# Cluster scores with the tokens stationary and the 16 centroids moving, written straight in token order

## The chip, the cores and the metric

One NeuronCore of a Trainium2 chip runs the whole program. The time is the device time of that core for one launch, in microseconds; the kernel before was run three times: 958.29, 959.78 and 960.33 us, median 959.78 us. All profile rows below come from one profiled execution of it.

## The reference

Three stages, in fp32. The change is in the first.

```python
q_n = q / (norm(q) + 1e-6); k_n, c_n the same            # B=2, H=8, S=768, D=64
q_assign = argmax(einsum('bhsd,hcd->bhsc', q_n, c_n), -1)  # 16 centroids per head
k_assign = argmax(einsum('bhsd,hcd->bhsc', k_n, c_n), -1)
mask = q_assign[..., :, None] == k_assign[..., None, :]
scores = where(mask, q @ k.T / sqrt(D), -1e9)
attn = softmax(scores); x = (attn @ v) -> (1536, 512)
x = moe(x)        # top-1 of 8 experts, 512 -> 1024 -> 512, gated
out = moe2(x)     # 512 -> 2048 -> 512 with a clamped square
```

The length of a token does not change its argmax, so the kernel scores unnormalised tokens against normalised centroids. To keep fp32 accuracy with matmuls in the faster fp32r form, an operand is split into a high part (fp32r) and a low part (the rest).

## The kernel before, in words

The 16 heads (2 x 8, called 0 to 15) run one after the other through a software pipeline; each head has 6 tiles of 128 queries and 6 of 128 keys. Every engine has its own program in fixed order (blocks `block.tensor`, `block.scalar`, `block.vector`, `block.gpsimd`, `block.sync`), and semaphores tie them together; no scheduler moves anything. On each engine `attend(h)` has six steps `s` = 0 to 5. Heads 0 and 1 get their operands in a prologue before the first `attend`; for a head h+2 they are made inside `attend(h)`.

For one head, in the order of the data:

- GpSimd writes each token twice side by side (L355, `dup`), TensorE transposes the tiles into PSUM (`operands`, L1059), ScalarE copies them to `qk_t` as high parts (L499), VectorE writes the low parts (L733 for q, L738 for k). `qk_t` has four groups of six tiles: A1 (q high, in both halves of the partitions), A2 (q low in partitions 0 to 63), B1 (k: high above, low below), B2.
- GpSimd copies the head's centroids from `cen_t` to `cst` (`place_centroids`, L373 and L374).
- **Cluster scores** (`cluster_scores`, L1063 to L1074): `cst` is the stationary side, 64 columns wide, of which 16 hold centroids and the others zeros; 384 tokens move. Eight matmuls add up into one 64x384 PSUM area, whose partitions are (k or q, first or second half of the tiles, centroid). Rows alternate between 128 and 64.
- ScalarE copies this to SBUF (`copy_cluster_scores`, L513, 64x384), and TensorE transposes it back in three 128x128 pieces (`cluster_rows`, L1079), so that tokens are partitions and the scores of a token lie in its row.
- VectorE takes the maximum (L747), compares (L752), turns the comparison into a label (L758, L763) and the labels into one-hot rows (L769).
- TensorE transposes the one-hots (`onehots`, L1088), and ScalarE writes them to partitions 64 to 79 of A2 and B2 (L507). They make the mask part of the score matmul L1104.

Then come the score matmuls (L1103, L1104), row maximum (L780), exponential (L518), transposes of the probabilities (L1117), their high and low copies (L544 on ScalarE, L830 on VectorE), the product with v (L1131, L1133), and the transposes of the outputs (L1145) which VectorE normalises (L806).

TensorE does `cluster_scores(h + 2)` at step 5 of `attend(h)`, ahead of that step's probability transposes, and `cluster_rows(h + 2)` behind them. VectorE does L747 and L752 at step 5, L758 at its end, L763 and L769 at step 0 of `attend(h + 1)`; TensorE wants the one-hots in step 1 of `attend(h + 1)`. While it runs the attention, GpSimd has little to do; behind it come four large subtractions for the first expert's weights (L342).

Of the kernel before, what the change touches and what calls it, by code (L numbers as in the profile page):

```python
# [26 lines left out]
F32 = mybir.dt.float32  # L27
F32R = mybir.dt.float32r
# [7 lines left out]
P = 128  # L36
BANK = 512
B, H, S, D = 2, 8, 768, 64
NC = 16
BH = B * H  # L40
QT = S // P
# [35 lines left out]
def build(nc, q, k, v, centroids, w_gate, w_ogate, w1, w2, w_in, w_out, out):  # L77
# [8 lines left out]
    def place(name, shape, dt, at=None):  # L86
        size = 4 if dt != BF16 else 2
        for n in shape[1:]:
            size *= n
        size = -(-size // 32) * 32  # L90
        if at is None:
            at, cursor[0] = cursor[0], cursor[0] + size
        else:
            at[0], at = at[0] + size, at[0]
        return nc.alloc_sbuf_tensor_at(name, list(shape), dt, offset=at)
# [55 lines left out]
    cst = place("cst", [P, 2, 4, 6 * NC], F32R, small)  # L151
    ct_sb = place("ct_sb", [P, GW], F32, small)
# [37 lines left out]
    with ctx:  # L190
        ps = ctx.enter_context(nc.psum_tensor("ps", [P, 8, BANK], F32))

        def sem(name):
            return ctx.enter_context(nc.semaphore(name))
# [14 lines left out]
        ct_done, ct_copied, cs_done, cl_done = sem("ct_done"), sem("ct_copied"), sem("cs_done"), sem("cl_done")  # L209
# [33 lines left out]
        cs_ps = ps[:, 7, 0:GW].rearrange("p (t n) -> p t n", n=P)[:, :, 0:4 * NC]\  # L243
            .rearrange("p t (a c) -> p t a c", c=NC)
        ct_ps = ps[0:4 * NC, 7, 0:GW]
# [65 lines left out]
        def _(pool):  # L311
# [56 lines left out]
            def place_centroids(h, u):  # L368

                if h >= 2:  # L370
                    pool.wait_ge(ct_done, h - 1)
                c = slice(h % H * NC, (h % H + 1) * NC)
                pool.tensor_copy(cst[:, u, 0:2, 2 * NC:3 * NC], cen_t[:, 0:2, c])  # L373
                pool.tensor_copy(cst[:, u, 2:4, 3 * NC:4 * NC], cen_t[:, 1:3, c]).then_inc(cst_done, 1)  # L374
# [113 lines left out]
        def _(act):  # L488
# [22 lines left out]
            def copy_cluster_scores(h):  # L511
                act.wait_ge(ct_done, h + 1)
                act.activation(ct_sb[0:4 * NC], ct_ps, ACT.Copy).then_inc(ct_copied, 1)  # L513

# [14 lines left out]
            def attend(h, u, first, ahead):  # L529
                un = 1 - u  # L530
                for s in range(QT):
# [3 lines left out]
                    if s == 5 and ahead >= 2:  # L535
                        copy_cluster_scores(h + 2)
# [23 lines left out]
            copy_cluster_scores(0)  # L560
# [8 lines left out]
            copy_cluster_scores(1)  # L569
# [119 lines left out]
        def _(dve):  # L689
            dve.memset(onehot[:], 0.0)  # L690
            dve.memset(x_sb[:, :, :, DM:], 0.0)
# [26 lines left out]
            dve.memset(ct_sb[4 * NC:], 0.0)  # L718
# [321 lines left out]
        def _(pe):  # L1040
# [22 lines left out]
            def cluster_scores(h, u):  # L1063


                pe.wait_ge(opd_done, 4 * h + 4)
                pe.wait_ge(cst_done, h + 1)
                for a in range(2):
                    cols = slice(2 * NC * (1 - a), 2 * NC * (1 - a) + 4 * NC)
                    for j, (rows, t) in enumerate(((P, A1), (D, A2), (P, B1), (D, B1))):  # L1070
                        tiles = qk_t[0:rows, u, t + a * HALF:t + (a + 1) * HALF, :].rearrange("p t n -> p (t n)")
                        last = mm(ct_ps, cst[0:rows, u, j, cols], tiles, start=(a == 0 and j == 0),  # L1072
                                  stop=(a == 1 and j == 3))
                last.then_inc(ct_done, 1)  # L1074

            def cluster_rows(h):
                pe.wait_ge(ct_copied, h + 1)
                for t in range(HALF):
                    last = tr(x_ps[:, t * P:(t + 1) * P], ct_sb[:, t * P:(t + 1) * P], ident[:])  # L1079
                last.then_inc(cs_done, 1)  # L1080
# [68 lines left out]
            def attend(h, u, first, ahead):  # L1149
                un = 1 - u  # L1150
                for s in range(QT):
# [8 lines left out]
                    if s == 5 and ahead >= 2:  # L1160
                        cluster_rows(h + 2)
# [28 lines left out]
            cluster_rows(0)  # L1190
# [9 lines left out]
            cluster_rows(1)  # L1200
# [189 lines left out]
```

## Time and profile before

| | |
|---|---|
| runs | 958.29, 959.78, 960.33 us |
| span of the profiled execution, first to last instruction | 959.3 us |
| prologue of the attention (to the first `attend`) | about 38 us |
| one head in the steady loop | 20.66 us |
| attention ends | about 367 us |
| TensorE busy | 853.2 us, 89% |
| VectorE, ScalarE, GpSimd busy | 543.7, 382.0, 320.2 us |

The profiled execution's own time is its span of 959.3 us and what lies around it, and this agrees with the runs to within 1 us. The time of a head is the distance of two cluster score blocks in the chain of waits (219.81 less 199.15). "PE" in the rows is TensorE's matmul side, "PEld" its load of the stationary side, DVE VectorE, ACT ScalarE, POOL GpSimd. A line of the timeline gives start and length of a group of equal instructions; in brackets how long the engine was idle before it and who ended that. The chain of waits goes back from the last instruction of the program and names what each moment of the span was waiting for. The matmul clock is shown as a share of 2.4 GHz, so that 0.50 is 1.2 GHz.

### The profile page before, as it was taken

The numbers are of one execution on the slowest core, as the hardware profiler recorded it, in microseconds if no ns is written. First come the engines' busy times: TensorE is split into PE (matmuls) and PEld (weight loads), VectorE is DVE, ScalarE is ACT, GpSimd is POOL, SyncE is SP. The second block draws the span as 40 slices with busy tenths as digits, with TensorE's granted clock in tenths as the row PEclk, the third lists the DMA queues.
The fourth block names the chain that finished last, engine by engine and source line by source line (L and its number), as shares of the span: only waits on it lengthen the run. The fifth ranks groups of instructions, "written<-read, shape, count | busy, mean of one in ns | idle before, by whom it ended". The sixth has DMA issues, their size and how long they took to land.

```text
span 959.3 us, 13920 instructions
## 1 busy us (share of the span) xinstructions
PE 853.2 (89%) x4379; PEld 691.9 (72%) x4380; DVE 543.7 (57%) x862; ACT 382.0 (40%) x762; POOL 320.2 (33%) x302
## 2 busy tenths in 40 slices
PE   4899999999999973389997997999699999999995
PEld 2687777777777762278776876877588888888884
DVE  4487787787778786134445345343744544454442
ACT  2577677777677751021211221122122332232222
POOL 4222222222322274448874664666400010001001
PEclk9799999999999997599999999999899999999998
DMA  8000000100000065698996696786300010001001
GB/s 269 25 26 25 26 25 25 49 25 25 25 25 8 0 219 181 217 261 264 329 339 240 206 332 218 230 319 219 99 1 0 1 45 1 1 1 44 1 1 44
DMA packets 46388, 105.23 MB, mean 110 GB/s; under 512 B 6545, under 2 KB 12689, under 8 KB 45329
## 3 DMA queue, kind: packets, MB, share of 16 engines
q1 hardware_dynamic: 24656, 51.48, 16.0%
q0 software_dynamic: 17408, 48.26, 15.0%
q10 hardware_dynamic: 4288, 5.03, 1.9%
q8 instruction: 20, 0.33, 0.1%
q14 instruction: 16, 0.12, 0.0%
HBM read 98.45 MB, written 6.32 MB: 109 GB/s over the span
## 4 chain that ended last, share of the span: by engine, by line
PE 70%; DVE 13%; DMA 6%; issue 5%; ACT 3%; POOL 2%; DVEq 1%; ACTq 1%
PE ps L1343 14%; PE ps L1330 14%; PE ps L1290 8%; PE ps L1270 7%; PE ps L1117 5%; DMA x_in<-sorted_rows 5%; PE ps L1072 4%; DVE coef L962 4%; PE ps L1103 3%; PE ps L1133 2%; PE ps L1104 2%; PE ps L1145 2%; PE ps L1131 2%; PE ps L1059 2%; PE ps L1088 2%
## 5 line engine op out<-in xcount | busy, mean ns | idle before, releaser
L342 POOL TENSOR_TENSOR weights<-staging,weights 128x2048 fp32r<-128x2048 f32 x38 | 174.9, 4612 | 38.4 <-DMA weights<-in_moe_w 30.2
L1343 PE MATMUL ps<-weights,g_t 128*128 128x512 f32 x576 | 145.0, 401 | 9.0 <-DVE g_t L1033 9.0
L1330 PE MATMUL ps<-y_t,weights 128*128 128x512 f32 x576 | 141.5, 395 | 0.0
L1343 PEld LDWEIGHTS ps<-weights,g_t 128*128 128x128 f32 x576 | 108.7, 190 | 35.9 <-DVE g_t L1033 10.1
L1330 PEld LDWEIGHTS ps<-y_t,weights 128*128 128x128 f32 x576 | 108.2, 188 | 25.7
L1290 PE MATMUL ps<-weights,h_t 128*128 x456 | 114.5, 409 | 3.9 <-issue 3.8
L830 DVE TENSOR_TENSOR p_t<-ps,p_t 128x384 fp32r<-128x384 f32 x192 | 99.9, 548 | 31.4 <-ACT p_t L544 30.2
L1270 PE MATMUL ps<-weights,x_t 128*128 x456 | 111.3, 401 | 2.0 <-DVE x_t L956 1.7
L1290 PEld LDWEIGHTS ps<-weights,h_t 128*128 128x128 f32 x456 | 87.9, 196 | 24.6 <-issue 6.0
L1270 PEld LDWEIGHTS ps<-weights,x_t 128*128 128x128 f32 x456 | 85.6, 191 | 20.6 <-issue 2.6
L480 POOL DMA_INDIRECT out<-y_sb,token_u x12 | 11.9, 995 | 255.8 <-ACT y_sb L676 253.6
L780 DVE TENSOR_REDUCE nmax<-ps 128x1 f32<-128x768 f32 x96 | 90.9, 946 | 6.4 <-PE ps L1104 5.3
L544 ACT ACTIVATE p_t<-ps 128x384 fp32r<-128x384 f32 x192 | 84.0, 490 | 22.2 <-PE ps L1117 21.3
L662 ACT ACTIVATE g_a<-g_a,half 128x512 f32<-128x512 f32 x48 | 34.7, 724 | 143.7 <-DVE g_a L1026 142.2
L518 ACT ACTIVATE prob<-ps,nmax 128x768 f32<-128x768 f32 x96 | 87.2, 909 | 7.6 <-DVE nmax L780 7.3
L1117 PE MATMUL ps<-ident,prob 128*128 128x128 f32 x576 | 83.0, 281 | 2.5 <-ACT prob L518 0.8
L1103 PE MATMUL ps<-qk_t 128*128 128x384 f32 x192 | 75.9, 395 | 1.4 <-ACT qk_t L507 1.1
L1117 PEld LDWEIGHTS ps<-ident,prob 128*128 128x128 f32 x576 | 66.1, 143 | 12.3 <-DVE p_t L830 7.0
L1026 DVE TENSOR_SCALAR g_a<-ps 128x512 f32<-128x512 f32 x48 | 33.1, 689 | 72.1 <-PE ps L1330 72.1
L1133 PE MATMUL ps<-p_t,v_s 128*128 128x384 f32 x192 | 65.6, 341 | 4.5 <-DVE x_sb L806 4.3
L617 ACT ACTIVATE h_t<-ps 128x1024 fp32r<-128x1024 f32 x19 | 19.5, 1027 | 125.0 <-PE ps L1280 101.8
L1104 PE MATMUL ps<-qk_t 80*128 80x384 f32 x192 | 67.2, 350 | 0.0
(144 smaller groups left out, 1159.5 us busy)
## 6 DMA issues: line engine op xcount, KB each, us to landing
weights<-in_moe_w POOLq DMA_DIRECT2D x32, 1024.0 KB, 8.4
staging<-in_moe_w SPq DMA_DIRECT2D x32, 1024.0 KB, 6.3
x_in<-sorted_rows ACTq DMA_DIRECT2D x19, 258.0 KB, 5.1
weights<-in_moe_w_in POOLq DMA_DIRECT2D x4, 1024.0 KB, 8.1
staging<-in_moe_w_in SPq DMA_DIRECT2D x4, 1024.0 KB, 5.6
staging<-in_moe_w_out SPq DMA_DIRECT2D x4, 1024.0 KB, 5.8
weights<-in_moe_w_out POOLq DMA_DIRECT2D x4, 1024.0 KB, 7.2
raw<-in_q SPq DMA_DIRECT2D x16, 192.0 KB, 2.7
```

What stands on the lines that cost most here:

```text
L342: pool.tensor_tensor(weights[:, unit % 2, 1, c * CHUNK:(c + 1) * CHUNK], staging[:, n % 2, :], hi.bitcast(F32), ALU.subtract).then_inc(w_r ...
L518: act.activation(prob[:, c, :].rearrange("p (a n) -> p a n", a=2), s_ps[c % 2], ACT.Exp, bias=nmax[:, c % 2:c % 2 + 1], accum_out=sums[:, ...
L780: dve.tensor_reduce(nmax[:, c % 2:c % 2 + 1], s_ps[c % 2], AX.XY, ALU.max, negate=True)\
L830: dve.tensor_tensor(p_t[:, s % 2, 1, t], pt_ps[:, t], p_t[:, s % 2, 0, t].bitcast(F32), ALU.subtract).then_inc(ptl_done, 1)
L1103: mm(o, qk_t[:, u, A1 + c, :], b1, start=True, stop=False)
L1104: last = mm(o, qk_t[0:D + NC, u, A2 + c, :], b2, start=False, stop=True)
L1117: last = tr(ps[:, 4 + t, c * P:(c + 1) * P], prob[:, HALF * g + c, k:k + P], ident[:])
L1133: last = mm(ot_ps, v_s[:, u, k, :], p_t[:, s % 2, 0, t, :], start=(k == 0), stop=(k == QT - 1))
L1270: last = mm(ps[:, n, :], x_t[:, u, a, k, :], flat[:, bass.ds(base + (b * UNIT + w), BANK)], start=(k == 0 and j == 0), stop=(k == KC - 1 a ...
L1290: last = mm(ps[:, 5 + u, :], h_t[:, a, n, :], flat[:, bass.ds(base + (b * UNIT + w), DM)], start=(n == 0 and j == 0), stop=(n == FC - 1 an ...
L1330: last = mm(ps[:, 4 + n % 2, :], wi[:, a, k, f * P:(f + 1) * P], y_ts[g % 2][:, b, k, :], start=(k == 0 and j == 0), stop=(k == KC - 1 and ...
L1343: last = mm(ps[:, t, :], g_t[:, n % 2, a, t * P:(t + 1) * P], wo[:, b, f, :], start=(f == 0 and j == 0), stop=(f == FC2 - 1 and j == 2))
```

## The change

The sides are exchanged. For each of the 6 tiles and each of q and k, the tile of 128 tokens is loaded as the stationary side, and the 16 centroid columns move over it, once for the high part and once for the low part: 24 matmuls of 128x16 in place of 8 of 64x384. The result has tokens in partitions at once, so the ScalarE copy and the three transposes go, with their semaphores. The A2 and low matmuls use 80 rows (`D + NC`) where the one before used 64; rows 64 to 79 of A2 hold one-hots, or at first nothing, so VectorE zeroes them once at the start (16 partitions x 1536 elements), and `cst` has zeros there. `cst` shrinks to 16 columns per part, and GpSimd fills it with four copies of 16 columns in place of two of 2 x 16. VectorE's own five steps stay as they are.

```diff
-    cst = place("cst", [P, 2, 4, 6 * NC], F32R, small)
-    ct_sb = place("ct_sb", [P, GW], F32, small)
+    cst = place("cst", [P, 2, 4, NC], F32R, small)
...
-        cs_ps = ps[:, 7, 0:GW].rearrange("p (t n) -> p t n", n=P)[:, :, 0:4 * NC]\
-            .rearrange("p t (a c) -> p t a c", c=NC)
-        ct_ps = ps[0:4 * NC, 7, 0:GW]
+        cs_ps = ps[:, 7, 0:2 * QT * NC].rearrange("p (t a c) -> p t a c", a=4, c=NC)
...
             def place_centroids(h, u):
                 if h >= 2:
-                    pool.wait_ge(ct_done, h - 1)
+                    pool.wait_ge(cs_done, h - 1)
                 c = slice(h % H * NC, (h % H + 1) * NC)
-                pool.tensor_copy(cst[:, u, 0:2, 2 * NC:3 * NC], cen_t[:, 0:2, c])
-                pool.tensor_copy(cst[:, u, 2:4, 3 * NC:4 * NC], cen_t[:, 1:3, c]).then_inc(cst_done, 1)
+                pool.tensor_copy(cst[:, u, 0, :], cen_t[:, 0, c])
+                pool.tensor_copy(cst[0:D, u, 1, :], cen_t[0:D, 1, c])
+                pool.tensor_copy(cst[:, u, 2, :], cen_t[:, 1, c])
+                pool.tensor_copy(cst[0:D, u, 3, :], cen_t[0:D, 2, c]).then_inc(cst_done, 1)
...
-            def copy_cluster_scores(h):
-                act.wait_ge(ct_done, h + 1)
-                act.activation(ct_sb[0:4 * NC], ct_ps, ACT.Copy).then_inc(ct_copied, 1)
...
             dve.memset(onehot[:], 0.0)
+            dve.memset(qk_t[D:D + NC, :, A2:A2 + QT, :].bitcast(F32), 0.0)
...
-            dve.memset(ct_sb[4 * NC:], 0.0)
             dve.memset(cst[:].bitcast(F32), 0.0).then_inc(cen_ev, 1)
...
                 pe.wait_ge(opd_done, 4 * h + 4)
                 pe.wait_ge(cst_done, h + 1)
-                for a in range(2):
-                    cols = slice(2 * NC * (1 - a), 2 * NC * (1 - a) + 4 * NC)
-                    for j, (rows, t) in enumerate(((P, A1), (D, A2), (P, B1), (D, B1))):
-                        tiles = qk_t[0:rows, u, t + a * HALF:t + (a + 1) * HALF, :].rearrange("p t n -> p (t n)")
-                        last = mm(ct_ps, cst[0:rows, u, j, cols], tiles, start=(a == 0 and j == 0),
-                                  stop=(a == 1 and j == 3))
-                last.then_inc(ct_done, 1)
-
-            def cluster_rows(h):
-                pe.wait_ge(ct_copied, h + 1)
-                for t in range(HALF):
-                    last = tr(x_ps[:, t * P:(t + 1) * P], ct_sb[:, t * P:(t + 1) * P], ident[:])
+                for n in range(QT):
+                    for j, parts in enumerate((((P, 0, A1), (D + NC, 1, A2)), ((P, 2, B1), (D + NC, 3, B1)))):
+                        for rows, part, at in parts:
+                            last = mm(cs_ps[:, n % HALF, 2 * (n // HALF) + j, :], qk_t[0:rows, u, at + n, :],
+                                      cst[0:rows, u, part, :], start=(part == 2 * j), stop=(part == 2 * j + 1))
                 last.then_inc(cs_done, 1)
```

The calls of `copy_cluster_scores` (three on ScalarE) and `cluster_rows` (three on TensorE) go too.

TensorE's program in step 5 of a head, before: `qk_t` are the tokens, `cst` the centroids, `prob` the probabilities, `ct_sb` the copied scores.

```order
L1133 MATMUL ps<-p_t,v_s 128x384
L1072 MATMUL ps<-qk_t,cst 64x384 x8
L1117 MATMUL ps<-ident,prob 128x128 x6
L1079 MATMUL ps<-ident,ct_sb 128x128 x3
L1103 MATMUL ps<-qk_t 128x384
```

And in the changed kernel, at the same place:

```order
L1117 MATMUL ps<-p_t,v_s 128x384
L1062 MATMUL ps<-cst,qk_t 128x16 x24
L1101 MATMUL ps<-ident,prob 128x128 x6
L1087 MATMUL ps<-qk_t 128x384
L1088 MATMUL ps<-qk_t 128x384
```

The block keeps its place ahead of the probability transposes (now L1101); the three transposes behind them are gone.

VectorE's program at the start, before (`cen` are the raw centroids):

```order
L690 MEMSET onehot 128x768
L691 MEMSET x_sb 128x12x4
L692 MEMSET half 128x1
L694 TENSOR_TENSOR cen<-cen 128x64
...
L716 TENSOR_TENSOR cen_s<-cen_u,cen_s 128x128
L718 MEMSET ct_sb 64x384
L719 MEMSET cst 128x768
L721 TENSOR_TENSOR back_w<-ident 128x8x64
L724 CAST cen_t<-ps 128x384
```

And after the change:

```order
L681 MEMSET onehot 128x768
L682 MEMSET qk_t 16x2x768
L683 MEMSET x_sb 128x12x4
L684 MEMSET half 128x1
L686 TENSOR_TENSOR cen<-cen 128x64
...
L708 TENSOR_TENSOR cen_s<-cen_u,cen_s 128x128
L710 MEMSET cst 128x128
L712 TENSOR_TENSOR back_w<-ident 128x8x64
L715 CAST cen_t<-ps 128x384
```

A memset of 1536 elements per partition stands ahead of the centroid work; behind it 1152 elements of memset have become 128.

## Rows read from the trace of the kernel before

**Rows 1.** The page: busy time of the engines, and TensorE's clock by slices.

```profile
PE 853.2 (89%) x4379; PEld 691.9 (72%) x4380; DVE 543.7 (57%) x862; ACT 382.0 (40%) x762; POOL 320.2 (33%) x302
PEclk9799999999999997599999999999899999999998
```

**Rows 2.** Chain of waits through one head: start us, us, what.

```profile
199.15 2.43 PE ps L1072 x8
201.58 0.49 PE ps L1117 x3
202.09 0.50 ACT p_t L544
...
203.09 0.35 DVE cmax L747
...
219.81 2.43 PE ps L1072 x8
```

**Rows 3.** Timeline, same place and a head earlier: start us, us, engine, line, operation.

```profile
186.97 0.55 PE L1088 MATMUL ps<-ident,onehot 128*128 128x128 f32 x3 [1.05 <-DVE onehot L769]
...
198.99 2.59 PE L1072 MATMUL ps<-qk_t,cst 128*64 128x384 f32 x8
201.51 0.88 PE L1117 MATMUL ps<-ident,prob 128*128 128x128 f32 x6
201.62 0.48 ACT L513 ACTIVATE ct_sb<-ps 64x384 f32<-64x384 f32 x1 [2.48 <-PE ps L1072]
202.22 0.49 PE L1079 MATMUL ps<-ident,ct_sb 128*128 128x128 f32 x3
202.62 0.56 DVE L830 TENSOR_TENSOR p_t<-ps,p_t 128x384 fp32r<-128x384 f32 x1 [1.86 <-ACT p_t L544]
```

**Rows 4.** Chain of waits, one head earlier: L1145 (80 columns move), transposes L1088, score matmul L1104.

```profile
188.17 0.63 PE ps L1145 x6
188.80 0.33 PE ps L1088 x3
...
189.30 0.18 PE ps L1104
```

**Rows 5.** Stationary loads by line: ns min/median/max, first and last start, forms.

```profile
L1072 PEld LDWEIGHTS ps<-qk_t,cst x128: 129/132/182, 12.0 to 325.2; 128*64 128x64 f32 x64, 64*64 64x64 f32 x64
L1145 PEld LDWEIGHTS ps<-back_w,o_t x192: 186/192/192, 52.3 to 366.2; 128*128 128x128 f32 x192
L1225 PEld LDWEIGHTS ps<-hot,ones x12: 104/104/144, 371.9 to 372.2; 128*128 128x128 bf16 x12
```

**Rows 6.** Timeline of the prologue.

```profile
1.06 0.70 DVE L690 MEMSET onehot<- 128x768 f32 x1 [0.91 <-PEq L1380]
2.54 0.23 DVE L694 TENSOR_TENSOR cen<-cen 128x64 f32<-128x64 f32 x1 [0.72 <-DMA cen<-in_centroids]
4.45 1.72 DVE L711 TENSOR_SCALAR cen_u<-cen,cen_n 128x64 f32<-128x64 f32 x1
4.50 1.62 POOL L355 COPY dup<-raw 128x768 f32<-128x768 f32 x2
12.02 4.15 PE L1072 MATMUL ps<-qk_t,cst 128*64 128x384 f32 x8 [1.18 <-DVE qk_t L738]
18.31 0.36 DVE L747 TENSOR_REDUCE cmax<-ps 128x12 f32<-128x192 f32 x1 [6.35 <-PE ps L1079]
```

**Rows 7.** Chain of waits in the prologue: start us, us, what.

```profile
17.64 0.65 PE ps L1079 x3
```

**Rows 8.** One stretch: us, busy of PE, PEld, DVE, ACT, POOL, clock, DMA share, GB/s.

```profile
32.05:45.70 13.65, 12.90 (x43) 9.44 (x44) 6.51 (x14) 6.03 (x13) 3.17 (x6) 0.50 0.14 44
```

**Rows 9.** Timeline in head 14, and VectorE's line L785 over the program.

```profile
339.30 4.54 POOL L342 TENSOR_TENSOR weights<-staging,weights 128x2048 fp32r<-128x2048 f32 x1
339.39 4.49 DVE L785 TENSOR_SCALAR rsum<-sums 128x6 f32<-128x6 f32 x1
...
L785 DVE TENSOR_SCALAR rsum<-sums x16: 159/161/4492, 51.7 to 359.7; 128x6 f32<-128x6 f32 x16
```

More of the change, by code:

```diff
@@ L208, in build @@
         b2_done, vs_done, vhi_done = sem("b2_done"), sem("vs_done"), sem("vhi_done")
-        ct_done, ct_copied, cs_done, cl_done = sem("ct_done"), sem("ct_copied"), sem("cs_done"), sem("cl_done")
+        cs_done, cl_done = sem("cs_done"), sem("cl_done")
         cst_done = sem("cst_done")
@@ L534, in attend @@
                         copy_operand(h + 2, BATCH_OF[s], u, False)
-                    if s == 5 and ahead >= 2:
-                        copy_cluster_scores(h + 2)
                     if s == 1 and ahead >= 1:
@@ L559, in _ @@
                 copy_operand(0, b, 0, True, FIRST_BANKS[0][b])
-            copy_cluster_scores(0)
             for b in range(2):
@@ L568, in _ @@
             copy_operand(1, 3, 1, True, FIRST_BANKS[1][3])
-            copy_cluster_scores(1)
             expo(0, 2, 0)
@@ L1159, in attend @@
                     transpose_probs(h, s, first)
-                    if s == 5 and ahead >= 2:
-                        cluster_rows(h + 2)
                     if s == 0 and ahead >= 2:
@@ L1189, in _ @@
                 operands(1, b, (opd_done, b + 1), bank=FIRST_BANKS[1][b])
-            cluster_rows(0)
             onehots(0, 0, None)
@@ L1199, in _ @@
             scores(0, 3, 0, True)
-            cluster_rows(1)
             attend(0, 0, True, 2)
```

## The prediction

> **What bounds the kernel now.** I read the page first: TensorE is busy for 853.2 us of a 959.3 us span, no other engine for more than 57%, and after the start its clock is at full speed through the whole attention [rows 1]. That share does not say what a change in the cluster step is worth, so I took the chain of waits through one head of the loop [rows 2]. It shows a ring with two halves. From the one-hots to the end of the next cluster score block the chain runs over TensorE without a gap; from there it runs over the first three probability transposes, the ScalarE copy of `p_t`, and then VectorE's steps (maximum L747 to one-hots L769) until TensorE can transpose the one-hots. In the second half TensorE works ahead and then waits for VectorE, 1.05 us in each head [rows 3]. The head takes 219.81 - 199.15 = 20.66 us [rows 2]. So what counts in the loop is the length of the score block itself and of VectorE's half; TensorE time spent between the block and the one-hots is covered by that wait.
>
> The timeline then shows which of the removed pieces are in the ring [rows 3]. The score block is: it goes from 198.99 to 201.51, 2.52 us for 8 matmuls. The ScalarE copy is not: it ends at 201.62 + 0.48 = 202.10, when the copy of `p_t` starts, which the chain says was waiting for the transposes (L1117), not for the copy [rows 2, 3]. The three transposes L1079 are not either: they run at 202.22 to 202.71, while VectorE is busy with `p_t` from 202.62 on and comes to the maximum only at 203.09. They take TensorE's time behind the block, where it is going to wait anyway.
>
> **The change, part by part, in the loop.** This concerns heads 2 to 15, 14 heads.
>
> Removed: the 8 matmuls, 2.52 us of the ring. The copy (0.48 us of ScalarE) and the transposes (0.49 us as the timeline has them, 3 x 0.11 = 0.33 us at their spacing) [rows 3, 4] give back nothing: the copy is hidden by the transposes L1117, the others by the 1.05 us wait, which grows to about 1.2 us. If the 1.05 us cover were absent, they would be worth 0.33 us a head.
>
> Added: 24 matmuls whose stationary side is 128 columns wide and whose moving side is 16. No row shows exactly this. With so short a moving side the load of the stationary side should set the pace. The load rows show 132 ns for the 64 columns of L1072 and 192 ns for 128 fp32 columns (L1145), so 64 more columns cost about 60 ns and 128 about 120 at most, behind a fixed part that overlaps [rows 5]. The nearest row at work is L1145, with 128 fp32 columns to load and 80 to move: 0.63 us for 6, 105 ns each; the transposes L1088 take 0.33 us for 3, 110 ns [rows 4]. I take 110 ns: 24 x 0.110 = 2.64 us. Bounds: below, the bf16 loads of L1225 start within 0.3 us for 12, 27 ns apart [rows 5], so 24 x 0.027 = 0.65 us, which would be 1.9 us less than before; above, the pace of L1072 itself, 2.52/8 = 0.315 us [rows 3], where each load waits for the matmul ahead: of it 0.16 us is the 384 columns at 2.4 GHz, and 0.155 stays for a short matmul, so 24 x 0.155 = 3.7 us. I stay near L1145, because 128 columns in a 4-byte type are what its load does too; the bf16 row loads half the bytes, and in 104 ns where this type needs 192.
>
> So the block grows by 2.64 - 2.52 = 0.12 us, and a first load of 192 ns where 132 stood adds a few hundredths [rows 5]: +0.13 us a head, all in the ring, since everything behind it (transposes, `p_t`, VectorE's half) starts that much later. 14 x 0.13 = +1.8 us.
>
> The Trainium skill bears on this in two places. "TensorE: Matmul & The Clock Gate", section LDWEIGHTS, says that a load takes its columns divided by 1.2 per ns whatever the rows: 53 ns for 64 columns and 107 for 128. The 60 ns between the two load rows agree, and the block would be 24 x 0.107 = 2.57 us, +0.05 us a head, by an estimate from that page. "TensorEngine Tiling (Array Packing)", section When to Use Tiling, advises the opposite of this change: where the moving side has 64 columns or fewer, swap the sides. The kernel before was the swapped form. Its Key Properties say that a change of the tiling mode drains the array, which fits 0.315 us for matmuls that alternate between 128 and 64 rows, against 0.18 us for L1104, which moves as many columns [rows 4].
>
> GpSimd's centroid copies go from two to four per head. The rows that bear on it are TensorE's and VectorE's waits, none of which is for them; they are made a head ahead, and I count 0. VectorE reads the same 192 scores per partition from the same bank in another order, 0.35 us as before [rows 2], so 0 there as well.
>
> **The prologue.** Heads 0 and 1 have their cluster step with little to hide it, at the low clock (1.2 GHz), so here removed parts do count.
>
> At the very start VectorE gets a memset of 1536 elements per partition, twice that of L690 (0.70 us), so 1.35 us, and it had 0.72 us of idle time ahead of the centroid work [rows 6]: that work starts 0.6 us later. Its tail stretched over the GpSimd copy L355 (L711 took 1.72 us, ending at 6.17, as L355 did at 6.12), so part of the 0.6 us is absorbed by less of that stall, or else more of the small steps fall into it. Behind it 1152 elements of memset become 128, which gives back 0.9 us ahead of `cen_t`. The sum is between -0.65 us (delay absorbed) and +0.1 us (not absorbed); I take -0.2.
>
> Head 0's block begins at 12.02 and VectorE's maximum at 18.31, 6.29 us later, since the block (4.15 us), the ScalarE copy, six other transposes and L1079 stand between [rows 6]. With 24 matmuls at the low clock, where L1079 takes 0.65/3 = 0.217 us [rows 7], the block is 5.2 us and the maximum follows at once, with 0.25 us for the last one to drain: 5.45 us. That is -0.8 us. Head 1 likewise loses its ScalarE copy and transposes but has 1.1 us more of block; its first transposes of probabilities gain nothing more, and I count 0. Together the prologue gives -1.0 us by its end.
>
> From 32.05 to 45.70 us the clock is at 1.2 GHz [rows 8]. If it rises at the same moment as before while the work is 1.0 us further on, that much more work is done at half speed, and half the gain is lost. I count -0.8 us.
>
> **Sum.** +1.8 - 0.8 = +1.0 us. The profiled execution's 959.3 us would become 960.3; the runs' median stands 0.5 us above its span, so 960.8 us.
>
> **The rivals.** A difference of under 0.2% (1.9 us) can't be told from none for this kernel, whose three runs span 2.0 us.
>
> R1, loads faster than L1145's. If loads of `qk_t` tiles go at a pace between the bf16 row's and mine, say 0.08 us, the block is 1.9 us, -0.6 us a head, 14 x 0.6 = 8.4 us, and with 0.8 us in the prologue 950.6 us; at the bf16 row's own 27 ns it would be 14 x 1.9 = 26 us. For it: short moving sides, and fp32r is not the fp32 of L1145. Against it: the 192 ns of the load row [rows 5], for the type of equal width. 7%.
>
> R2, slower than before: loads that don't overlap. In L1072 each load started only when the matmul ahead was through [rows 3], 0.155 us beyond its columns. If the new block has this too (its stationary rows alternate between 128 and 80), it takes 3.7 us, +1.2 us a head, 14 x 1.2 = 16.8, less 0.5 in the prologue: 976 us. It decides as soon as the pace passes 0.125 us, where the loop costs 14 x 0.5 = 7 us. For it: the row of L1072. Against: L1145 keeps 105 ns [rows 4], and L1104, whose 80 rows alternate with the 128 rows of L1103, takes 0.18 us for 384 columns, so the step from 128 to 80 rows costs no such stop. 7%. A fall of the clock in the loop, since the block now moves 384 columns where it moved 3072, belongs to the same case: a low stretch as long as a fifth of the 13.65 us of [rows 8] after each block would cost 1.4 us a head, 20 us in all. Against it: TensorE stays occupied during the block, and transposes in rows leave the clock up. 3%.
>
> R3, the collision at the end. In head 14 VectorE's L785, normally 0.16 us, waits 4.49 us because GpSimd's L342 started 0.09 us ahead of it [rows 9]. Both hang on the same one-hots, so the distance should stay, but if VectorE comes first, 4.3 us go: 956.5 us. 10%.
>
> R4, the clock in the prologue. If the denser block of head 1 or the earlier work brings the rise at 45.70 forward by a quarter of the 13.65 us [rows 8], 3.4 us of work at half speed become 1.7: 959.1 us, 13%. Later by as much gives 962.5 us, 10%.
>
> That leaves 50% for my forecast as it stands: 960.8 us, with 959.5 to 962.3 as its own range.
>
> **How the numbers follow.** Faster by over 0.2% means under 957.9 us: R1, R3 and a small part of R4 (0.02), 0.19. Slower by over 0.2% means over 961.7: R2 with its clock case (0.10), most of the late clock (0.07), and the upper edge of my own case (0.11), 0.28. The rest, 0.53, is the same within 0.2%. The range must reach to R3's 956.5 and somewhat above the late clock: 956.2 to 963.4 us, which leaves out R1, R2 and little else.
>
> **What would show it.** In the new trace the 24 matmuls are one block of 2.6 to 2.7 us; loads of 190 ns, starting 0.11 us apart; the distance of two blocks is 20.8 us; TensorE's wait for the one-hots is longer than 1.05 us. The maximum of head 0 comes 5.45 us behind the start of its block. A block under 2.4 us or over 2.9 us makes the step wrong on which the sign in the loop rests; a head below 20.6 us with a block of 2.6 would mean that the copy or the transposes had been in the ring after all.

## The result, and the profile after

The changed kernel takes **967.67 us** (median of four runs, 964.8 to 972.45) against 960.06 us of the kernel before in the same session. The ratio is 1.0084, 95% interval 1.0054 to 1.0113: slower by 7.6 us, where 960.8 us and a range of 956.2 to 963.4 were predicted. The profiled execution below is the slowest of the four, so its sums are made against its own span of 970.7 us; the kernel before has 959.3 us.

First the page of the changed kernel, TensorE's busy time and clock, to be read against [rows 1].

```profile
PE 866.4 (89%) x4587; PEld 730.3 (75%) x4588; DVE 538.0 (55%) x862; ACT 375.8 (39%) x746; POOL 323.9 (33%) x334
PEclk9999999989999997599999899899899999999998
```

TensorE is busy for 13 us more, and in the clock row there are a few 8s where [rows 1] had 9. In the slices this shows weakly, since one slice is 24 us. The next view is the chain of waits through one head of the changed loop (start us, us, what), the counterpart of [rows 2].

```profile
137.99 2.69 PE ps L1062 x24
140.67 0.42 PE ps L1101 x3
141.11 0.50 ACT p_t L537
...
158.83 2.67 PE ps L1062 x24
```

The ring is the same as before: block, three transposes, `p_t`, and then VectorE's half. The head takes 158.83 - 137.99 = 20.84 us where it took 20.66. The same view, three heads on:

```profile
201.74 3.13 PE ps L1062 x24
204.87 1.39 PE ps L1101 x6
206.26 0.32 PE ps L1087
...
224.50 2.69 PE ps L1062 x24
```

This head takes 22.76 us. The six transposes behind the block need 1.39 us and a score matmul 0.32 us, where [rows 4] have 0.18 us for one: these are the durations of 1.2 GHz. Next the loop of the changed kernel from head 2's block to head 15's, and two short stretches of it: the busy time of each engine (PE, PEld, DVE, ACT, POOL), then TensorE's clock, DMA share and GB/s:

```profile
53.00:330.00 277.00, 264.60 (x1797) 237.90 (x1795) 207.68 (x418) 196.43 (x443) 73.18 (x183) 0.95 0.08 25
57.00:60.40 3.40, 3.40 (x15) 3.11 (x14) 2.73 (x7) 1.79 (x5) 0.00 (x0) 0.50 0.00 0
203.80:210.60 6.80, 6.80 (x30) 6.51 (x30) 3.18 (x8) 2.81 (x6) 0.00 (x0) 0.50 0.00 0
```

And the loop of the kernel before:

```profile
54.00:323.00 269.00, 254.12 (x1631) 208.97 (x1630) 208.13 (x418) 201.58 (x457) 70.60 (x158) 1.00 0.08 25
```

Before, the clock was at 2.4 GHz for the whole loop (1.00). Now it is at 1.2 GHz in seven stretches of it, 57.0 to 60.4, 77.5 to 80.9, 162.8 to 166.2, 183.3 to 186.7, 203.8 to 210.6, 227.7 to 231.1 and 313.0 to 316.4 (27.3 us), and in an eighth right behind head 15's block, 333.5 to 336.9 (30.7 us in all). TensorE is busy for the whole of the two shown (3.40 of 3.40 and 6.80 of 6.80 us). Each begins 2.2 to 4.2 us behind the start of a score block. TensorE was not idle ahead of the fall either: here are the 3.7 us from the start of head 2's block to the first fall, and the same 3.7 us of a head that keeps its clock.

```profile
53.30:57.00 3.70, 3.70 (x34) 3.70 (x33) 1.82 (x3) 0.65 (x4) 1.66 (x7) 1.00 0.02 7
137.80:141.50 3.70, 3.70 (x34) 3.68 (x33) 1.82 (x3) 0.58 (x3) 1.66 (x7) 1.00 0.00 0
```

The new block itself is close to what was predicted. Its loads over the whole program (ns min/median/max, first and last start):

```profile
L1062 PEld LDWEIGHTS ps<-cst,qk_t x384: 186/189/338, 12.3 to 332.6; 128*128 128x128 f32 x192
```

In the loop, at 2.4 GHz, the first and the last of 24 loads start 2.56 us apart, 0.111 us from one to the next. By the rule in "TensorE: Matmul & The Clock Gate", section LDWEIGHTS, of the Trainium skill (columns divided by 1.2 per ns) an estimate for 128 columns is 107 ns; at this clock the trace agrees to 4%. At 1.2 GHz it does not: in head 0's block, here by its loads alone, they start 0.213 us apart and take 333 ns in the rows instead of 189.

```profile
L1062 PEld LDWEIGHTS ps<-cst,qk_t x24: 286/333/333, 12.3 to 17.1; 128*128 128x128 f32 x12, 80*128 80x128 f32 x12
```

A third piece lies behind the attention. Two loads of sorted rows, issued by ScalarE, and the first MoE transposes that wait for them; the kernel before, then the changed one:

```profile
394.68 1.48 ACTq L596 DMA_DIRECT2D x_in<-sorted_rows  x2
397.56 1.08 PE L1250 MATMUL ps<-ident,x_in 128*128 128x128 f32 x4 [25.12 <-DMA x_in<-sorted_rows]
```

```profile
398.76 0.97 POOL L435 DMA_INDIRECT sorted_rows<-x_sb,slot_u  x1 [0.30 <-issue]
402.98 3.19 ACTq L587 DMA_DIRECT2D x_in<-sorted_rows  x2
407.36 1.08 PE L1230 MATMUL ps<-ident,x_in 128*128 128x128 f32 x4 [27.02 <-DMA x_in<-sorted_rows]
```

From the last scatter to the first MoE matmul it was 6.72 us and is now 407.36 - 398.76 = 8.60 us, and 1.71 us of the difference lies in the issue of the two loads (3.19 against 1.48). In that gap the DMA queues of the changed kernel show one packet of code:

```profile
q14 instruction: 1, 0.01, 0.6%
```

The kernel before has none in its gap.

**Where the profiled 11.4 us are.** Head 2's block begins at 53.26 us instead of 54.64: -1.4. From there to head 15's block it takes 276.79 us instead of 268.34, +8.45: 13 x 0.17 = 2.2 for the longer block, and 6.2 in the heads with a low clock (27.3 us of it). From head 15's block to the attention's end +0.85, with two low stretches (333.5 to 336.9 and 354.0 to 357.4) where the kernel before has one (346.1 to 349.5). The router's gap +1.9. Behind the first MoE matmul +1.6, where the changed execution has one low stretch of 3.4 us more; this one comes and goes between executions of it.

### The profile page after: what moved, and what is told of

The parts are those of the page before. It is cut to its first block, busy times and chain, and to the rows that moved or that the text cites. A ratio compares the mean times of both kernels' runs of the same rounds, so it can differ in the third digit from the quotient of the medians.

```text
span 970.7 us, 14340 instructions
## 1 busy us (share of the span) xinstructions
PE 866.4 (89%) x4587; PEld 730.3 (75%) x4588; DVE 538.0 (55%) x862; ACT 375.8 (39%) x746; POOL 323.9 (33%) x334
## 4 chain that ended last, share of the span: by engine, by line
PE 75%; DVE 11%; DMA 5%; issue 4%; ACT 3%; POOL 2%; DVEq 1%; ACTq 0%
PE ps L1323 14%; PE ps L1310 14%; PE ps L1270 8%; PE ps L1250 8%; PE ps L1101 6%; PE ps L1062 5%; DMA x_in<-sorted_rows 5%; DVE coef L953 3%; PE ps L1087 3%; PE ps L1117 3%; PE ps L1088 3%; PE ps L1115 3%; PE ps L1129 2%; PE ps L1050 2%; PE ps L1072 2%
## 5 line engine op out<-in xcount | busy, mean ns | idle before, releaser
L1101 PE MATMUL ps<-ident,prob 128*128 128x128 f32 x576 | 87.2, 291 | 3.6 <-DVE p_t L821 1.5
L1101 PEld LDWEIGHTS ps<-ident,prob 128*128 128x128 f32 x576 | 70.9, 150 | 11.4 <-DVE p_t L821 8.0
L1087 PE MATMUL ps<-qk_t 128*128 128x384 f32 x192 | 78.0, 406 | 1.4 <-ACT qk_t L506 1.1
L1117 PE MATMUL ps<-p_t,v_s 128*128 128x384 f32 x192 | 68.5, 357 | 4.5 <-DVE x_sb L797 4.4
L1088 PE MATMUL ps<-qk_t 80*128 80x384 f32 x192 | 69.1, 360 | 0.0
```

The costliest lines, as they stand in the source:

```text
L1087: mm(o, qk_t[:, u, A1 + c, :], b1, start=True, stop=False)
L1088: last = mm(o, qk_t[0:D + NC, u, A2 + c, :], b2, start=False, stop=True)
L1101: last = tr(ps[:, 4 + t, c * P:(c + 1) * P], prob[:, HALF * g + c, k:k + P], ident[:])
L1117: last = mm(ot_ps, v_s[:, u, k, :], p_t[:, s % 2, 0, t, :], start=(k == 0), stop=(k == QT - 1))
```

## The experiments

Four questions were open: whether the clock falls because of the new block's few moving columns, whether the copy and the transposes had really been free, what the block of before spent its 0.315 us per matmul on, and why two loads take longer. The diffs below are excerpts.

**128 columns move.** The changed kernel, but each token tile meets the 16 centroids eight times side by side; only the first 16 results are used.

```diff
-    last = mm(cs_ps[:, n % HALF, 2 * (n // HALF) + j, :], qk_t[0:rows, u, at + n, :],
-              cst[0:rows, u, part, :], start=(part == 2 * j), stop=(part == 2 * j + 1))
+    o = 64 * n + NC * (2 * a + j)
+    last = mm(ps[:, 7, o:o + 8 * NC].rearrange("p (r c) -> p r c", c=NC),
+              qk_t[0:rows, u, at + n + HALF * a, :],
+              cst[0:rows, u, part, :].unsqueeze(1).broadcast_to([rows, 8, NC]), ...)
```

> The changed kernel, but 128 columns move per matmul of the score block (the 16 centroids eight times over) instead of 16; the spare results are overwritten by the next group. The load of the stationary side (0.11 us) stays longer than 128 columns at 2.4 GHz (0.053 us), so the block should keep its 2.6 to 2.7 us. Theory A (the clock falls in the attention because the block lets so few columns through the array): the eight low stretches between 57 and 337 us go or nearly so, a head takes 20.83 us throughout, attention ends 5 to 6 us earlier than in the changed kernel, and the time is 961 to 963 us. Theory B (the clock falls for the pattern of 24 short load and matmul pairs, whatever moves): the low stretches stay, 966 to 969 us. Theory C (the loss is not the clock but the block's length): the block would be no shorter, and the time stays at 966 to 969 us with or without the low stretches.

Measured: 961.59 us (960.36 to 963.0, 12 runs), ratio 1.0024 (1.0008 to 1.0039). Chain of waits, two blocks, and the whole loop as a stretch:

```profile
176.10 2.72 PE ps L1063 x24
...
196.94 2.73 PE ps L1063 x24
```

```profile
51.30:321.80 270.50, 253.31 (x1796) 226.02 (x1794) 207.63 (x417) 194.60 (x444) 73.08 (x183) 1.00 0.08 25
```

Eight times the columns, and the head is as long (20.84 us) while the loop's clock is at 1.00 again. So the length of the block is set by the loads, and the low stretches come from what the matmuls move and not from the work around the block: theory A holds, B and C do not. It is not chance of one profile: the two kernels with 128 moving columns further down also have 1.00 in these 270.5 us. Between this kernel and the changed one 6 to 8 us lie in the medians; in the profiles 6.3 us is in the loop (270.5 against 276.8), and head 2's block begins 2 us earlier, since head 0's block takes 3.36 us instead of 5.30. All three kernels with 128 moving columns have such a short first block (2.91 to 3.36 us), those with 16 and 48 do not (5.30 and 5.33); why was not tested.

Where the 6.3 us come from can be read from TensorE's side. In the loop it is busy for 264.60 us in the changed kernel and for 253.31 us here, 11.3 us more, and it waits less for VectorE. Its waits for the one-hots and for `p_t` (total us, times, longest) in the changed kernel, then in this one:

```profile
PE ps L1072 <- DVE onehot L760: 9.7, 11, 1.1
PE ps L1101 <- DVE p_t L821: 1.2, 6, 0.2
```

```profile
PE ps L1075 <- DVE onehot L760: 13.6, 13, 1.1
PE ps L1104 <- DVE p_t L821: 2.3, 12, 0.2
```

The waits shrink by 5.0 us, and 11.3 - 5.0 = 6.3 us is what the loop grows by: nearly half of the time that TensorE loses at 1.2 GHz is taken out of its waits.

**48 columns move.** The same with 3 in place of 8.

> The same with 48 moving columns (the centroids three times over). Theory A: fewer low stretches than with 16, not necessarily none; 961 to 967 us. Theory B and C: as with 16, 966 to 969 us.

Measured: 966.28 us (963.32 to 968.01, 9 runs), ratio 1.0063 (1.0042 to 1.0084). Four low stretches in the loop, 13.7 us, one of them:

```profile
139.40:142.80 3.40, 3.40 (x15) 3.11 (x14) 2.68 (x6) 1.79 (x5) 0.00 (x0) 0.50 0.00 0
```

From the third block on, heads outside them take 20.83 us, the others 21.38 to 22.0. The time of 966.28 us fits theories A, B and C alike; it is the trace that decides. Its low clock lies between, as it should if the moved columns are the cause: 30.7 us of low clock with 16 columns, 13.7 with 48 (one profile), none with 128. This kernel and the one with 128 columns differ in nothing but the columns.

**The changed kernel again,** to see whether the low stretches are chance.

> The changed kernel once more, for a second profile of it. Theory A says that a low stretch follows a score block by chance of how the two line up, so number and places of the low stretches should differ from the first profile (9 x 3.4 us in the loop), the undisturbed heads should again take 20.83 us, and the time should be 964 to 972 us. If the loss were in fixed places, the same heads would be the long ones again.

Measured: 969.85 us (963.85 to 972.38, 10 runs), ratio 1.0093 (1.0067 to 1.0119). The slowdown is confirmed. That the stretches would lie elsewhere was wrong: they lie at the same eight places to 0.1 us, as this one, which answers to 203.80 to 210.60 above:

```profile
203.70:210.50 6.80, 6.80 (x29) 6.51 (x30) 2.88 (x7) 2.51 (x6) 0.00 (x0) 0.50 0.00 0
```

What makes some heads keep the clock and others lose it, with the same program, was not settled. Both profiles are of slow executions for this kernel (972.45 and 970.99 us, where its fastest took 963.85); whether those that were not profiled have the same eight places is not shown.

**Without the copy and the transposes.** The kernel before, without `copy_cluster_scores` and `cluster_rows`. The labels are read from what stands in PSUM without them, so this kernel leaves out that part of the computation; the number of operations behind it is the same.

```diff
-                    if s == 5 and ahead >= 2:
-                        copy_cluster_scores(h + 2)
...
-                    if s == 5 and ahead >= 2:
-                        cluster_rows(h + 2)
```

> The kernel before with the ScalarE copy and the three transposes left out, and nothing in their place: VectorE reads whatever lies in the bank, so the labels and all that follows are not the reference's; only the attention's times are read. Theory F (these pieces were hidden in the loop): a head takes 20.66 us as before, TensorE's wait for the one-hots grows from 1.05 to about 1.35 us, and only the prologue gains, about 2 us at head 0 and 1 to 2 us at head 1. Rival G (they were in the ring): a head of 20.2 to 20.35 us.

Measured: 958.48 us in one run. Head 2's block begins 3.8 us earlier by the chain (51.05 instead of 54.87), as expected for the prologue. Little of it arrives at the end; 1.7 us of it goes in the two loads of sorted rows, which take 3.16 us here. Chain of waits, and TensorE's two waits in that head:

```profile
174.63 2.44 PE ps L1065 x8
195.30 2.44 PE ps L1065 x8
```

```profile
200.14 0.87 PE L1104 MATMUL ps<-ident,prob 128*128 128x128 f32 x6 [0.19 <-DVE p_t L823]
...
203.80 0.55 PE L1075 MATMUL ps<-ident,onehot 128*128 128x128 f32 x3 [1.05 <-DVE onehot L762]
```

The head stays at 20.67 us: theory F holds and G does not, the copy and the transposes had been hidden. But the wait for the one-hots, which I had expected to grow (to 1.2 us in the prediction, to 1.35 above), stays at 1.05. TensorE now waits 0.19 us at the next probability transposes for `p_t`, and it starts everything behind them no earlier than before. The changed kernel shows the same two rows:

```profile
143.00 0.87 PE L1101 MATMUL ps<-ident,prob 128*128 128x128 f32 x6 [0.18 <-DVE p_t L821]
...
146.65 0.55 PE L1072 MATMUL ps<-ident,onehot 128*128 128x128 f32 x3 [1.05 <-DVE onehot L760]
```

**80 rows in place of 64.** The kernel before, whose 64-row matmuls take 16 rows more, on which the centroids are zero; the tokens' rows 64 to 79 of A2 are zeroed once by GpSimd, which also copies the centroids in four pieces as in the changed kernel. Still 8 matmuls of 384 columns, with copy and transposes.

```diff
-   for j, (rows, t) in enumerate(((P, A1), (D, A2), (P, B1), (D, B1))):
+   for j, (rows, t) in enumerate(((P, A1), (D + NC, A2), (P, B1), (D + NC, B1))):
```

> The kernel before (centroids stationary, copy and transposes kept), but its matmuls that used 64 rows use 80, with zeros in the centroid tile there; GpSimd zeroes rows 64 to 79 of the low q tiles in its idle time. Theory D (what made the old block slow is the step between 128 and 64 rows, 0.14 us each): the eight matmuls go at the 0.18 us of L1104, the block takes 1.42 us in place of 2.52, a head 19.56 us in place of 20.66, the prologue loses 3 us, and the time is 941 to 945 us. Rival E (the 0.315 us come from the 64-column stationary side or from the small output): the block stays at 2.5 us and the time at 958 to 961 us.

Measured: **942.54 us** (939.63 to 945.08, 5 runs), ratio 0.9819 (0.9787 to 0.9851). Loads and blocks: the timeline of the kernel before (two of its eight loads; the bracket is the idle time of the loading side), then the timeline and the chain of this one.

```profile
178.31 0.13 PEld L1072 LDWEIGHTS ps<-qk_t,cst 128*64 128x64 f32 x1 [0.15 <-issue]
...
178.62 0.13 PEld L1072 LDWEIGHTS ps<-qk_t,cst 64*64 64x64 f32 x1 [0.19 <-issue]
```

```profile
188.47 1.25 PEld L1077 LDWEIGHTS ps<-qk_t,cst 128*64 128x64 f32 x8
```

```profile
188.65 1.45 PE ps L1077 x8
208.23 1.46 PE ps L1077 x8
```

From the first load to the last it is 1.11 us, where it was 2.22. The second load starts 0.055 us behind the first and each one after it 0.175 us behind the one ahead, the pace of the score matmuls in [rows 4], where they started 0.316 to 0.320 us apart; between the loads no idle time is listed any more. The head takes 19.58 us, 1.08 less. So nearly half of each matmul's time in the old block, 0.14 of 0.32 us, went with the step from 128 rows to 64 and back.

**Half of it.** Only the q part has 80 rows, the k part keeps 64.

> The padded kernel with only the q matmul of the low part at 80 rows, the k one at 64 again: of the eight matmuls' steps between 128 and 64 rows half are left, four and the way out. Theory D: 8 x 0.18 + 4 x 0.14 = 2.0 us for the block, a head 20.1 us, half way between 20.66 and 19.58. Rival E: no such proportion.

Measured: 950.3 us in one run, the head 192.28 - 172.19 = 20.09 us by the chain:

```profile
172.19 1.88 PE ps L1077 x8
...
192.28 1.89 PE ps L1077 x8
```

The block has four steps between 128 and 64 rows, the one behind it counted, where the kernel before has eight. Half of the steps, half of the gain, as expected.

**Another order.** The kernel before with its eight matmuls sorted: the four with 128 rows, then the four with 64. Nothing else differs, no row is padded.

```diff
+                n = 0
+                for j in (0, 2, 1, 3):
+                    rows, t = ((P, A1), (D, A2), (P, B1), (D, B1))[j]
+                    for a in range(2):
```

> The kernel before with the eight matmuls in another order: the four with 128 rows first, then the four with 64. Nothing padded, nothing zeroed. Theory D: only two steps are left, 8 x 0.18 + 2 x 0.14 = 1.7 us for the block, a head 19.85 us, 948 to 950 us. Rival H (matmuls with 64 rows are slow even one behind the other): the four of them keep 0.32 us each, the block takes 2.0 to 2.3 us, 953 to 957 us.

Measured: **946.09 us** (943.93 to 947.74, 4 runs), ratio 0.9868 (0.9828 to 0.9907). Chain of waits:

```profile
170.94 1.58 PE ps L1074 x8
...
190.77 1.58 PE ps L1074 x8
```

The head takes 19.83 us, 0.83 less, with the same matmuls and two steps: theory D holds, H does not. In the one step inside the block the load starts 0.44 us behind the one ahead and the next one 0.055 us behind it. The order alone costs 14 us of the program, 2 us more than the expected 948 to 950 us had it: 14 x 0.83 = 11.6 in the loop and the rest ahead of it, where the blocks of heads 0 and 1 take 3.01 us instead of 4.15. Counted by the head, a step costs 1.09 / 8 = 0.14 us with eight of them against none, and the kernels with four and two steps fit (0.57 and 0.83 us gained, 0.55 and 0.82 by this count).

**Both.** Sorted order for all heads, and 80 rows from head 2 on, when rows 64 to 79 have been written anyway, so that nothing has to be zeroed (the centroids are zero there).

```diff
+                low = D if isinstance(h, int) and h < 2 else D + NC
+                for j in (0, 2, 1, 3):
+                    rows, t = ((P, A1), (low, A2), (P, B1), (low, B1))[j]
```

> The kernel before with 80 rows in the loop (heads 2 to 15) as in the padded kernel, and for heads 0 and 1, where the padding needs the memset that held up the start by 1.1 us, 64 rows in grouped order and no memset. In the loop the 128-row matmuls also come first. A head takes 19.58 us, head 0's block starts at 12.0 us in place of 13.1 and is 0.3 to 0.6 us longer: 941 to 942 us, against 942.5 for the padded kernel.

Measured: 942.48 us (936.76 to 942.98, 6 runs), ratio 0.982 (0.9789 to 0.9851), heads of 19.57 to 19.62 us. It is the fastest measured here, together with the padded kernel; the memset that it saves at the start (its first block begins at 11.72 us instead of 13.14) does not show in the median.

**ScalarE's program as long as before.** The changed kernel with 128 moving columns, and a copy of 64x8 elements to an unused buffer wherever the score copy had stood.

```diff
+            def spare_copy(h):
+                act.wait_ge(cs_done, h + 1)
+                act.activation(spare[0:4 * NC], ident[0:4 * NC, 0:8], ACT.Copy)
```

> The changed kernel with 128 moving columns (so that the clock stays up in the loop), and on ScalarE, in each place where the kernel before copied the cluster scores, a wait for the same block and a copy of 64x8 elements between two small buffers whose result nobody reads. It asks where 1.9 us go behind the attention: the two loads of sorted rows on ScalarE took 1.48 us before and 3.19 after, and the first MoE matmul came 6.7 and 8.6 us behind the last scatter. Theory J (the removal of the copies moved ScalarE's program so that a piece of its code is fetched between those two loads): with the program as long as before at that point, the two loads take 1.5 us again, the first MoE matmul comes 6.7 to 7.0 us behind the last scatter, and the median falls by 1.8 us from the 961.6 us measured for the same kernel without the spare copies, to 959.8. Rival K (the loads are slow for another reason, such as when the attention ends or what VectorE and TensorE do): 3.2 us, 8.6 us and 961.6 us as there. Heads of 20.85 us by both.

Measured: 959.42 us (953.47 to 961.9, 12 runs), ratio 0.9992 (0.9969 to 1.0015). ScalarE's loads and the matmuls that wait for them:

```profile
390.33 0.96 POOL L436 DMA_INDIRECT sorted_rows<-x_sb,slot_u  x1 [0.30 <-issue]
394.41 1.48 ACTq L596 DMA_DIRECT2D x_in<-sorted_rows  x2
397.18 1.09 PE L1242 MATMUL ps<-ident,x_in 128*128 128x128 f32 x4 [25.27 <-DMA x_in<-sorted_rows]
```

1.48 us again, and 397.18 - 390.33 = 6.85 us from scatter to matmul. Theory J holds, K does not: with more instructions on ScalarE the loads are 1.64 us faster than in the same kernel without them (3.12 us). The medians go the same way, 959.42 us against 961.59, but they are of two sessions and their intervals touch (up to 1.0015 here, from 1.0008 there), so the 1.6 us rests on the traces.

**The spare copies in one place.** Nine of them together behind the attention, none inside it.

> The changed kernel with 128 moving columns, and on ScalarE nine spare copies of 64x8 elements (each with a wait that has long been met) together in one place behind the attention, ahead of the router's first exponential and so ahead of the two loads of sorted rows; none of them in the attention. Theory J (the place of the loads in ScalarE's program decides whether code is fetched between them): the two loads need 1.5 us as before the change, and the first MoE matmul comes 6.7 to 7.0 us behind the last scatter. Rival L (it is what ScalarE does during the attention that matters): 3.1 to 3.2 us and 8.6 us.

Measured: 957.86 us in one run.

```profile
394.47 1.48 ACTq L591 DMA_DIRECT2D x_in<-sorted_rows  x2
397.36 1.09 PE L1237 MATMUL ps<-ident,x_in 128*128 128x128 f32 x4 [25.42 <-DMA x_in<-sorted_rows]
```

So it is the number of instructions ahead of the loads and not what ScalarE does in the attention; L does not hold. The matmul comes 6.98 us behind the last scatter. The ten other profiles of the study fit: those with the score copy have 1.48 us, those without it and without spare copies 3.12 to 3.19. The code packets fit too. In the five profiles with slow loads one packet of queue q14 starts between the two loads (in the changed kernel at 403.55 us), in the other seven none does; both kernels with spare copies, which differ from the one with 128 columns on ScalarE alone, have it some 30 us ahead of the loads instead, at 363.17 and 364.01 us. "Runtime: NRT & Kernel Launch", section Instruction fetch mechanics, of the Trainium skill says that an engine's code comes in blocks of 256 instructions and that crossing from one to the next is mostly hidden. Here it was not: 1.7 us, on the path to the first expert.

## Why the prediction was wrong

Each step against what was measured:

| step | predicted | measured |
|---|---|---|
| a head of the loop, clock at 2.4 GHz | +0.13 us, 14 x = +1.8 | +0.17 us, 14 x = +2.4 |
| prologue | -0.8 us | -1.4 us |
| clock in the loop | stays up (97% for it) | 27.3 us at 1.2 GHz, +6.2 us |
| loads of sorted rows behind the attention | not considered | +1.7 to 1.9 us |
| copy and transposes | hidden | hidden |
| sum | +1.0 us | +7.6 us (median), +8.9 by the ratio of the second session |

The measured rows add up to +9.0 us. The first two were both missed by 0.6 us, in opposite directions, so that their sum of +1.0 us came out as predicted by luck. What moved the time out of the range is the clock in the loop, and behind it the loads of sorted rows, a term that the sum did not have.

**The step that failed** is in R2: "A fall of the clock in the loop, since the block now moves 384 columns where it moved 3072". I had it at 3%, on the ground that "TensorE stays occupied during the block, and transposes in rows leave the clock up". The first half is true by the profile's busy time and no reason: TensorE counts as busy in the low stretches as well. The second half compared with transposes, which move 128 columns for each 128 loaded, while the new block moves 16. The kernel with 128 columns is just that comparison, and it keeps the clock. No row of the kernel before had so short a moving side in a row of 24, so a bound from the traces was missing, and this called for a larger chance than 3%. Its price was too high as well: 1.4 us a head would need a low stretch in each head and half of the stretch lost. Seven stretches fell between the blocks of heads 2 and 15, and 6.2 us for their 27.3 us is under a quarter. It is not that the loads keep their pace: they go from 0.111 to 0.213 us. The stretches fall behind the block, where the ring runs over VectorE and TensorE has waits that shrink, 5.0 us of the 11.3 us by which its busy time grows.

**A second step that failed** is a term put at nothing without a reason: the prediction counts nothing behind the attention. The 1.7 to 1.9 us there, between the last scatter and the first MoE matmul, come from ScalarE's shorter program, as the two kernels with spare copies show.

**The size of the block** was right: 2.67 us in the chain against 2.43, a pace of 0.111 us against 0.110 assumed. One of the signs named in the prediction did not come: TensorE's wait for the one-hots stayed at 1.05 us, and TensorE waits 0.18 us for `p_t` instead. The head grew by 0.04 us more than assumed, 0.6 us in all.

**The prologue** gave 0.6 us more, and not by the terms assumed. VectorE's new memset of 1.34 us delayed the centroid work by 1.0 us and not 0.6. Rows of the changed kernel, to be read against [rows 6]:

```profile
2.11 1.34 DVE L682 MEMSET qk_t<- 16x1536 f32 x1 [0.36 <-issue]
...
3.53 0.22 DVE L686 TENSOR_TENSOR cen<-cen 128x64 f32<-128x64 f32 x1
...
4.66 1.41 DVE L695 TENSOR_TENSOR cen_n<-cen_n 128x1 f32<-128x1 f32 x1
...
12.28 5.29 PE L1062 MATMUL ps<-cst,qk_t 128*128 128x16 f32 x24 [1.18 <-DVE qk_t L729]
17.61 0.36 DVE L738 TENSOR_REDUCE cmax<-ps 128x12 f32<-128x192 f32 x1 [5.38 <-PE ps L1062]
```

The centroid work starts at 3.53 us where it was 2.54, and the instruction that stalls beside GpSimd's copy is now L695. By head 0's block 0.26 us of the delay is left, where I had -0.2. The maximum comes 5.33 us behind the start of the block, 5.45 predicted, and so 0.7 us earlier than in [rows 6]. Up to head 1's one-hots that gain stays (41.56 us, 42.32 before). Only there it doubles, by the chain of the changed kernel:

```profile
38.08 1.28 PE ps L1101 x6
...
41.56 0.56 PE ps L1072 x3
```

Six transposes still take 0.21 us each at 38.08; at 41.56 three take 0.19 each, as at 2.4 GHz. In the timeline the first score matmul at full speed starts at 40.04 (0.34 us, where the one at 37.55 has 0.52). Before, the clock came back at 45.70 [rows 8], and the same three one-hot transposes took 0.90 us. So R4's early case did occur: the slow part ends 5.7 us earlier, and that gave some 0.7 us of the 1.4, where I had priced 3.4 us at 1.7. That the gain comes from the clock is read from these rows; no run isolates it.

**The other rivals.** R1 did not happen: the token tiles' loads take 189 ns at 2.4 GHz, where L1145's took 192 [rows 5]. R3 did not either: in the changed kernel GpSimd's subtraction still starts first, by 0.08 us, and VectorE's L776 takes 4.51 us.

**What the prediction passed by.** It noted that the row alternation fits 0.315 us against 0.18 us, with a rule of the Trainium skill beside it ("TensorEngine Tiling (Array Packing)", Key Properties: a change of the tiling mode drains the array). The runs fit that for 128 against 64 rows, 0.14 us a step, and show no such cost between 128 and 80; that it is a drain which takes the time no run shows. The conclusion lay there and was not drawn: 1.1 us of the 2.5 us block was removable without swapping any sides. The same page's advice (When to Use Tiling, to swap and tile the columns where the moving side has 64 columns or fewer) fits in its first half, since the swapped form is 0.8% faster than the other as it stood and 2% once sorted; several tiles at once were not tried here.

## What to carry to other kernels

When a change replaces a few long matmuls by many short ones, count the columns that move beside the loads: a block that is equally long and equally busy can cost the clock of the work behind it. Before restructuring a block whose matmuls take longer than their columns, sort it by number of rows; that changes only an order, and here it gave 14 us where the restructuring lost 8. And a change that shortens an engine's program can move a fetch of its code into a critical place: look at code packets in any gap that grew without a reason.

## What the hardware showed that I had not expected

- The clock falls though TensorE is busy for 3.70 of the 3.70 us ahead of the fall and for 3.40 of 3.40 us behind it, and does so at the same eight places in two executions (to 0.1 us).
- Low clock from 53 to 337 us: 30.7 us with 16 moving columns, 13.7 us with 48, none with 128, at the same pace of loads (2.56 to 2.57 us for 24).
- Loads of the stationary side slow down with the clock: 0.111 us from one to the next at 2.4 GHz, 0.213 us at 1.2 GHz, for 128 columns.
- 27.3 us at 1.2 GHz cost the loop 6.2 us: TensorE is busy for 11.3 us more, and its waits give back 5.0 us.
- A step between 128 and 64 rows costs 0.14 us of the head: 20.66 us with eight steps, 20.09 with four, 19.83 with two, 19.58 with none. Steps between 128 and 80 rows show no such cost (loads 0.175 us apart).
- A fetch of code between two DMA issues of ScalarE costs 1.7 us; nine short copies with their waits, more or fewer, decide whether it falls there.
